# Clustered attention with two expert layers: who prepares the first two heads, and in which order

## What is computed

```python
q_assign = np.argmax(np.einsum('bhsd,hcd->bhsc', q_n, c_n), axis=-1)
k_assign = np.argmax(np.einsum('bhsd,hcd->bhsc', k_n, c_n), axis=-1)
mask = q_assign[:, :, :, None] == k_assign[:, :, None, :]
scores = scale * np.matmul(q, k.transpose(0, 1, 3, 2))
scores = np.where(mask, scores, -1000000000.0)
...
attn = attn / (np.sum(attn, axis=-1, keepdims=True) + 1e-09)
return np.matmul(attn, v).astype(np.float32)
```

## Time and profile before

| | us |
|---|---|
| median of 3 runs (839.62 to 842.99) | 840.84 |
| profiled execution | 838.19 |
| its span, first to last instruction | 836.4 |
| PE busy | 812.5 (97%) |
| DVE busy | 454.3 (54%) |
| ACT busy | 349.4 (42%) |
| POOL busy | 378.2 (45%) |

### The profile page before, as it was taken

One profiled execution on the slowest core, in us unless ns is written; L12 is line 12 of the kernel. 1 busy time (PEld: TensorE's weight loads), 2 busy tenths in 40 slices (PEclk: granted clock), 3 DMA queues, 4 the chain that ended last, 5 costly groups with the idle time before them and its releaser, 6 DMA issues.

```text
span 836.4 us, 13018 instructions
## 1 busy us (share of the span) xinstructions
PE 812.5 (97%) x4375; PEld 679.6 (81%) x4376; DVE 454.3 (54%) x685; ACT 349.4 (42%) x703; POOL 378.2 (45%) x323
## 2 busy tenths in 40 slices
PE   8999999999999899999999999999999999999995
PEld 4888898898898588888888888888888888888883
DVE  2969879879887779999877104531211121111110
ACT  1858678678687343334333443111212111121111
POOL 6997988988985255545545644000411011010001
PEclk8999999999999999999999999999999999999998
DMA  7444534534424287887767413300101000010001
GB/s 185 124 111 122 139 101 131 138 101 131 101 79 119 47 259 226 243 248 244 245 203 236 125 39 103 112 1 13 38 1 51 1 26 1 5 47 0 1 1 50
DMA packets 53114, 86.72 MB, mean 104 GB/s; under 512 B 22289, under 2 KB 24337, under 8 KB 53073
## 3 DMA queue, kind: packets, MB, share of 16 engines
q1 hardware_dynamic: 43920, 69.88, 29.3%
q0 software_dynamic: 3824, 11.29, 4.5%
q10 hardware_dynamic: 5328, 5.01, 1.8%
HBM read 73.29 MB, written 11.30 MB: 101 GB/s over the span
## 4 chain that ended last, share of the span: by engine, by line
PE 89%; POOL 5%; DVE 3%; issue 2%; DMA 1%; SPq 0%; ACT 0%; DVEq 0%; POOLq 0%
PE bank L1326 12%; PE bank L1328 12%; PE bank L1327 12%; PE bank L1419 8%; PE bank L1354 8%; PE bank L1228 6%; PE bank L1359 4%; PE bank L1423 4%; PE bank L1244 4%; PE bank L1212 3%; PE bank L1218 3%; PE bank L1246 3%; PE bank L1366 2%; PE bank L1257 2%; PE bank L1192 2%
## 5 line engine op out<-in xcount | busy, mean ns | idle before, releaser
L1159 DVE TENSOR_TENSOR ab_raw<-bank,a_sb 128x512 f32<-128x512 f32 x36 | 24.9, 691 | 195.2 <-PE bank L1328 189.3
L1007 DVE TENSOR_REDUCE neg_max<-bank 128x1 f32<-128x768 f32 x96 | 91.6, 954 | 40.5 <-PE bank L1218 39.6
L377 DVE TENSOR_TENSOR w_split<-stage,w_split 128x1024 fp32r<-128x1024 f32 x72 | 104.2, 1450 | 2.4
L761 ACT ACTIVATE pT_hi<-bank 128x384 fp32r<-128x384 f32 x192 | 84.9, 491 | 48.6 <-PE bank L1228 47.2
L373 DVE CAST w_split<-stage 128x1024 fp32r<-128x1024 f32 x68 | 66.0, 971 | 71.2 <-PE bank L1359 52.0
L978 DVE TENSOR_TENSOR pT_lo<-bank,pT_hi 128x384 fp32r<-128x384 f32 x192 | 97.5, 549 | 4.8 <-ACT pT_hi L761 4.8
L782 ACT ACTIVATE probs<-bank,neg_max 128x768 f32<-128x768 f32 x96 | 87.1, 908 | 11.6 <-DVE neg_max L1007 11.5
L655 POOL TENSOR_TENSOR hT_lo<-hT_raw,hT_hi 128x512 fp32r<-128x512 f32 x38 | 55.0, 1449 | 76.5 <-ACT hT_raw L830 76.0
L1228 PE MATMUL bank<-ident,probs 128*128 128x128 f32 x576 | 81.0, 275 | 1.8 <-ACT probs L782 1.1
L1419 PE MATMUL bank<-w_split,hT_hi 128*128 (+1 forms) x304 | 79.4, 403 | 0.5 <-issue 0.5
L886 ACT ACTIVATE a_sb<-bank 128x512 f32<-128x512 f32 x36 | 21.5, 598 | 139.0 <-PE bank L1328 139.0
(11 more groups left out here) (210 smaller groups left out, 1725.9 us busy)
## 6 DMA issues: line engine op xcount, KB each, us to landing
stage<-w SPq DMA_DIRECT2D x64, 512.0 KB
q_raw<-qT SPq DMA_DIRECT2D x32, 192.0 KB, 3.8
k_raw<-kT SPq DMA_DIRECT2D x32, 192.0 KB, 4.0
sorted_y<-y_sb ACTq DMA_DIRECT2D x19, 256.0 KB, 4.9
q_pair<-qT SPq DMA_DIRECT2D x8, 384.0 KB, 4.4
k_pair<-kT SPq DMA_DIRECT2D x8, 384.0 KB, 4.7
v_raw<-v_keys SPq DMA_DIRECT2D x16, 192.0 KB, 4.2
stage<-w_a SPq DMA_DIRECT2D x6, 512.0 KB
```

What stands on the lines that cost most here:

```text
L377: eng.tensor_tensor(dst[:, 1], stage[:, i % STAGES], dst[:, 0].bitcast(F32), ALU.subtract).then_inc(s_cv, 1)
L761: act.activation(pT_hi[:, half, part * GT:(part + 1) * GT, j * P:(j + 1) * P], pT_ps[part].rearrange("p (k q) -> p k q", q=P), ACT.Copy).t ...
L1007: dve.tensor_reduce(neg_max[:, qt % 2:qt % 2 + 1], scores[qt % 2][:, 0:S], AX_X, ALU.max, negate=True).then_inc(s_max, 1)
```

## The change

Only the work up to the first score of head 2 changes.

- ACT issues the four loads of head 0's rows, which SP issued before. Behind the square root ACT evaluates one exponential of a spare element and writes the identities of `back_w` from `ident`.
- `first_highs`: ACT writes the high parts `k_hl` and `q_hh` of heads 0 and 1, and for head 0 also the scaled q and the copy of k. `first_lows`: Pool keeps the low parts, and for head 1 the scaled q and the copy of k, on 64 partitions.
- Pool's iotas and selects stand ahead of its first wait for rows; the fills go to DVE, ahead of the centroids.
- The first pair's similarities go to two banks, six tiles each; DVE assigns the first half while PE multiplies the second, in two times five steps.
- PE transposes the one-hots twice, the second time shifted by two blocks (`one_hot` has two blocks more in front), so that head 0's rows come out in partitions 64 to 79 each time. ACT writes head 0's k mask and DVE its q mask straight to `k_hm` and `q_lm`; SP's mask DMAs for head 0 fall away, those for head 1 stay.
- Ahead of head 0's scores PE has 6 and 4 spins, where it had 9 and 14.
- Head 0's mask semaphore counts one pair less from then on; waits that are always met in the first pair are left out.

```diff
-        one_hot = sb("one_hot", [P, 4 * QT, 2 * C], BF16, att)
+        one_hot = sb("one_hot", [P, 2 + 4 * QT, 2 * C], BF16, att)
...
+        first_hot_T = bank[:, 6, :].bitcast(BF16)[:, 0:S]
+        first_sims = [bank[:, 7 - i, 0:2 * QT * C].rearrange("p (t c) -> p t c", c=C) for i in range(2)]
...
+        def load_rows(eng, g, slot):
+            for half in range(2):
+                rows = slice(half * D, half * D + D)
+                for raw, src in ((q_raw, qT), (k_raw, kT)):
+                    eng.dma_start(raw[rows, slot, :], src[bass.ds(g, 1)].rearrange("g d s -> (g d) s")).then_inc(s_qk[slot], 16)
...
             load_pair(0)
-            load_qk(0, 0)
             load_qk(1, 1)
...
             reload_pair(1)
-            mask(0, 0, 0)
             mask(1, 0, 1)
...
-            pool.memset(cen_pair[:, :, :, :], 0.0).then_inc(s_const, 1)
-            pool.memset(one_hot[:, :, :], 0.0).then_inc(s_const, 1)
             pool.iota(c_minus[:, :], pattern=[[1, C]], base=-C, channel_multiplier=0,
                       allow_small_or_imprecise_dtypes=True).then_inc(s_const, 1)
...
+            pool.wait_ge(s_set, 8)
+            pool.affine_select(out=tri[:, :], in_=tri[:, :], compare_op=ALU.is_ge, fill=0.0, base=0,
...
-            prepare(0, 0, 0)
-            prepare(1, 0, 1)
+            def first_lows(g):
+                q, k = q_raw[0:D, g], k_raw[D:P, g]
+                pool.wait_ge(s_khi, g + 1)
+                pool.tensor_tensor(k_hl[D:P, g], k, k_hl[D:P, g].bitcast(F32), ALU.subtract).then_inc(s_khl, 1)
+                pool.wait_ge(s_khl, g + 1)
+                pool.wait_ge(s_qs, g + 1)
+                pool.wait_ge(s_qhh, g + 1)
+                pool.tensor_tensor(q_lm[0:D, g], q, q_hh[0:D, g].bitcast(F32), ALU.subtract).then_inc(s_qlm, 1)
+                pool.wait_ge(s_qlm, g + 1)
+
+            pool.wait_ge(s_const, 17)
+            first_lows(0)
+            pool.wait_ge(s_qk[1], 64)
+            pool.wait_ge(s_khm, 1)
+            pool.tensor_tensor(k_hm[0:D, 1], k_raw[0:D, 1], one[0:D], ALU.mult).then_inc(s_khm, 1)
+            pool.wait_ge(s_qhh, 2)
+            pool.wait_ge(s_qs, 1)
+            pool.tensor_tensor(q_raw[0:D, 1], q_raw[0:D, 1], scale[0:D], ALU.mult).then_inc(s_qs, 1)
+            pool.wait_ge(s_khm, 2)
+            pool.wait_ge(s_qs, 2)
+            first_lows(1)
             split_v(0, 0, 0)
-            pool.memset(back_w[:, :, 0:D], 0.0).then_inc(s_const0, 1)
...
+            load_rows(act, 0, 0)
             act.wait_ge(s_csum, 1)
             act.activation(cen_n[:, 1:2], cen_n[:, 0:1], ACT.Sqrt).then_inc(s_csqrt, 1)
+            act.wait_ge(s_csqrt, 1)
+            act.activation(exp_spare[:, :], cen_n[:, 1:2], ACT.Exp, scale=0.0)
+            act.wait_ge(s_const, 1)
+            for half in range(2):
+                rows = slice(half * D, half * D + D)
+                act.activation(back_w[rows, :, 0:D], ident[rows, rows].unsqueeze(1).to_broadcast([D, G, D]), ACT.Copy).then_inc(s_bw, 1)
...
+            def first_highs(g):
+                act.wait_ge(s_qk[g], 64)
+                act.activation(k_hl[:, g], k_raw[:, g], ACT.Copy).then_inc(s_khi, 1)
+                act.activation(q_hh[:, g], q_raw[:, g], ACT.Copy, scale=float(D) ** -0.5).then_inc(s_qhh, 1)
+
+            first_highs(0)
+            act.wait_ge(s_qhh, 1)
+            act.activation(q_raw[0:D, 0], q_raw[0:D, 0], ACT.Copy, scale=float(D) ** -0.5).then_inc(s_qs, 1)
+            act.activation(k_hm[0:D, 0], k_raw[0:D, 0], ACT.Copy).then_inc(s_khm, 1)
+            first_highs(1)
...
             act.wait_ge(s_line, 4)
+            act.wait_ge(s_hotT, 1)
+            act.activation(k_hm[D:D + C, 0], hot_T[D:D + C, :], ACT.Identity, scale=mask_line[D:D + C, 0:1],
+                           bias=mask_line[D:D + C, 1:2]).then_inc(s_km0, 1)
             make_mask_rows(0)
...
+            for m, value in ((tri, 1.0), (before_e, 1.0), (rows_before_e, float(P)), (one_hot, 0.0), (cen_pair, 0.0),
+                             (ones, 1.0), (logits, 0.0)):
+                dve.memset(m[tuple([slice(None)] * len(m.shape))], value).then_inc(s_set, 1)
+            dve.memset(tile_thr[:, :, 0:1], -1.0).then_inc(s_set, 1)
...
             dve.tensor_scalar(cen_rows[:, :, :], cen_rows[:, :, :], cen_n[:, 7:8], None, ALU.mult).then_inc(s_cunit, 1)
-            dve.wait_ge(s_const, 5)
+            dve.wait_ge(s_const, 3)
+            dve.wait_ge(s_set, 8)
             dve.wait_ge(s_cT, 1)
-            for two in range(2):
-                rows = slice(two * D, two * D + D)
-                unit_T = bank[rows, 7, 0:P].rearrange("d (j two c) -> d j two c", two=2, c=C)[:, :, two, :]
-                for b in range(B):
+            for b in range(B):
...
-            for step in range(5):
-                assign(0, step)
+            for half in range(2):
+                n = 2 * QT
+                at = slice(half * n, half * n + n)
+                by_c = lambda v: v[:, at].unsqueeze(2).to_broadcast([P, n, C])
+                dve.wait_ge(s_sims0 if half == 0 else s_sims, 1)
+                dve.tensor_reduce(sim_max[:, at], first_sims[half], AX_X, ALU.max).then_inc(s_asgn, 1)
+                dve.wait_ge(s_asgn, 1 + 5 * half)
+                dve.tensor_tensor(sim_is_max[:, at, :], first_sims[half], by_c(sim_max), ALU.is_equal).then_inc(s_asgn, 1)
...
+                dve.tensor_tensor(one_hot[:, 2 + half * n:2 + half * n + n, 0:C], c_minus_ps[:, 0:n, :], by_c(first_idx),
+                                  ALU.is_equal).then_inc(s_asgn, 1)
+            dve.wait_ge(s_hotQ, 1)
+            dve.tensor_copy(q_lm[D:D + C, 0], first_hot_T[D:D + C, :]).then_inc(s_qm0, 1)
...
+            def first_similarities(half):
+                for t in range(QT):
+                    last = sim_rows(0, half * QT + t, first_sims[half][:, 2 * t:2 * t + 2, :])
+                last.then_inc((s_sims0, s_sims)[half], 1)
+
...
+            def first_hot_transposes():
+                pe.wait_ge(s_asgn, 10)
+                for out, back, done in ((hot_T, 2, s_hotT), (first_hot_T, 0, s_hotQ)):
+                    for t in range(QT):
+                        last = pe.transpose(out[:, t * P:(t + 1) * P],
+                                            one_hot[:, back + 4 * t:back + 4 + 4 * t, :].rearrange("p a c -> p (a c)"), ident_bf[:, :])
+                    last.then_inc(done, 1)
...
                     pe.wait_ge(s_qlm, g + 1)
                     pe.wait_ge(s_khm, g + 1)
-                    pe.wait_ge(s_mask[slot], (pp + 1) * 32)
+                    if slot == 1:
+                        pe.wait_ge(s_mask[1], (pp + 1) * 32)
+                    elif static(pp) and pp == 0:
+                        pe.wait_ge(s_qm0, 1)
+                        pe.wait_ge(s_km0, 1)
+                    else:
+                        pe.wait_ge(s_mask[0], pp * 32)
...
             pe.wait_ge(s_line, 6)
-            similarities(0, range(2 * QT))
-            spin(9)
-            hot_transposes(0)
-            spin(14)
+            pe.wait_ge(s_pair, 32)
+            pe.wait_ge(s_cTs, 2)
+            first_similarities(0)
+            first_similarities(1)
+            spin(6)
+            first_hot_transposes()
+            spin(4)
             over_pairs(pe, pair)
...
```

More of the change, by code:

```diff
@@ L416, in load_qk @@
             def load_qk(g, slot):
-                for half in range(2):
-                    rows = slice(half * D, half * D + D)
-                    sp.dma_start(q_raw[rows, slot, :], qT[bass.ds(g, 1)].rearrange("g d s -> (g d) s")).then_inc(s_qk[slot], 16)
-                    sp.dma_start(k_raw[rows, slot, :], kT[bass.ds(g, 1)].rearrange("g d s -> (g d) s")).then_inc(s_qk[slot], 16)
+                load_rows(sp, g, slot)
             def load_v(g, slot):
@@ new lines, in _ @@
+            pool.iota(row_no1[:, :, :], pattern=[[0, 1], [1, P]], base=1, channel_multiplier=0,
+                      allow_small_or_imprecise_dtypes=True).then_inc(s_const, 1)
+            pool.iota(place_no[:, :, :], pattern=[[P, T], [0, 1]], base=0, channel_multiplier=1,
+                      allow_small_or_imprecise_dtypes=True).then_inc(s_const, 1)
+            for m, pattern, step in ((row_no, [[0, 1], [1, P]], 0), (tile_row, [[0, 1], [P, TILES]], 0), (token_lane, [[0, 1]], 1),
+                                     (token_tile, [[1, T], [0, 1]], 0)):
+                pool.iota(m[tuple([slice(None)] * len(m.shape))], pattern=pattern, base=0, channel_multiplier=step,
+                          allow_small_or_imprecise_dtypes=True).then_inc(s_const, 1)
@@ L940, in _ @@
             dve.tensor_scalar(cen_rows[:, :, :], cen_rows[:, :, :], cen_n[:, 7:8], None, ALU.mult).then_inc(s_cunit, 1)
-            dve.wait_ge(s_const, 5)
+            dve.wait_ge(s_const, 3)
+            dve.wait_ge(s_set, 8)
             dve.wait_ge(s_cT, 1)
-            for two in range(2):
-                rows = slice(two * D, two * D + D)
```

(6 more changed lines are left out.)

97 lines of the change are left out of this document (44 added, 53 removed).

## The result

| | before | after |
|---|---|---|
| median, us (8 runs each) | 841.91 (838.67 to 843.87) | 835.12 (833.10 to 837.84) |
| profiled execution, us | 838.19 | 835.20 |
| its span, us | 836.4 | 833.5 |

The ratio is 0.9922, 95% interval 0.9898 to 0.9946: faster by 0.8%, 6.8 us between the medians. The two profiled executions differ by only 3.0 us. Both numbers need an explanation.

The account below looks back on a forecast made before the run. PE was taken to bound the kernel (97% busy), with Pool setting the pace up to head 2. First score 2.8 + wait 1.98 + clock 1.60 = 6.4 us, so 840.84 - 6.4 = 834.4 us, range 831.2 to 838.2.

Parts of the forecast that it names:

- the footing: Gain subtracted from the timed median 840.84 us, 2.65 above the profiled execution, rather than from the profiled 838.19.
- Term 1: Ahead of head 2: with Pool's queue shortened, PE's wait of 1.98 us goes.
- The spare time: At head 2, Pool was to be ready at least 4 us before PE needs it.
- Term 2: In head 2: PE stays busy from head 1, so the 1.60 us lost to the lower clock are gained.
- Term 3: First score of head 0: its second half starts at 17.2 instead of 20.02, 2.8 us gained (1.0 to 3.8).
- the start of the similarities: In the front, first pair: similarities start at 7.1 to 7.8, taken as 7.4, against 7.11 before.
- the pair's rows come late: Rival at the front: shared engines delay the first pair's rows, term 3 shrinks to 1.5, 835.7 us; chance 0.16.
- The steps of the assignment: DVE in the front: steps of 192 elements take 0.36 us each, five with gaps 1.95 us.
- Head 0's rows: Loads in the front: land not much later than 9.90; preparation done below 15 us, so not the bound.
- the signs of being wrong: Similarities past 8.5, ACT's mask activation past 18, clock 0.5 in head 0 or 1, PE wait over 1 us before head 3.
- Slower: the lower clock stays: Rival in heads 0 and 1: PE stays at 1.2 GHz, losing 0.48 us per us, 844.0 us; chance 0.06.

Follow-up runs that it names:

- constants alone: Kernel before with only Pool's constants moved ahead of its first wait, fills on DVE, back_w identities on ACT; 834.64 us, ratio 0.9933.
- before with more fillers: Kernel before with 26 instead of 14 filler spins on PE ahead of head 0's first score; 838.46 us, ratio 0.9974.
- rows on SP: Changed kernel with head 0's rows loaded by SP behind the first pair's rows instead of by ACT; 834.0 us, ratio 0.993.
- second profile of before: Kernel before, unchanged, profiled once more; 841.94 us, mean clock 0.986.
- the kernel with the gate weights late: Changed kernel with head 0's rows on SP, gate weights loaded behind the second pair's rows, 5 spins instead of 2 behind the centroid transpose; 836.65 us, ratio 0.9944.
- the changed kernel measured again: Changed kernel, unaltered, timed and profiled a second time; 835.19 us, ratio 0.993.
- front alone: Changed kernel with Pool's constants, fills and back_w put back on Pool, only the new front left; 834.51 us, ratio 0.9926.
- 16 fillers: Changed kernel with 16 spin matmuls instead of 2 behind the centroid transpose; 834.38 us, ratio 0.991.
- rows on SP and fillers: Changed kernel with head 0's rows on SP, 6 spins instead of 2 ahead of the similarities, 6 between the first score's halves; 834.42 us, ratio 0.9936.

## Why the prediction held, and where it did not

The forecast was 834.4 us (831.2 to 838.2), faster; measured 835.12. The direction is right and so are two of the three terms, but that the number is off by only 0.7 us is luck: the sum was 3.6 us too large (6.38 for the 2.79 of the profiles), and the footing was off by 2.9 us the other way (840.84 - 2.79 = 838.05 for 835.12).

- **Term 1, the wait ahead of head 2: right.** 1.98 us were foretold; the constants alone brought 1.98, the whole change 2.11. The spare time was 7.9 us, where "at least 4" was said. One step in its working is off: head 0 does not last to 33.79, which is the second score of head 1; head 1's first score stands at 29.94. The figure served as an upper bound only. And what Pool waited for at 29.19 was head 2's rows, not the scores of head 0.
- **Term 2, the clock in head 2: right.** 1.60 foretold, 1.55 in the profile, 1.61 with the constants alone, and 1.58 (17.91 - 16.33) in before with more fillers, where only PE came later and the wait was shorter.
- **Term 3, the first score: wrong in sign.** +2.8 foretold, -0.87 in the profile. The step that failed is the start of the similarities, 7.4, taken with the remark that a second queue brings little bandwidth: the pair landed at 10.64. The rival "the pair's rows come late" had this mechanism, with 7.4 to 9.5; an even share of the engines was not its worst case; head 0's loads were issued first and came ahead of the centroids as well, on which DVE starts at 4.44, 1.3 us later than before. By the rule cited from the Trainium skill, "DMA: Bandwidth & Descriptors", section "Queues, rings and completion order", a delay was to be expected, and the run agrees: 8.5 us from issue to landing beside ACT's loads, 3.9 with all on SP's queue. Of the 3.69 us by which the second half missed 17.2, this start is 3.33; about 1.0 of it is the late centroids (DVE is through with them at 8.39), the rest the pair's k. The steps from there on were right in sum, 10.16 us for 9.8: the similarities took 5.12 up to the first filler for 3.9, since they ran wholly at the lower level behind the wait of 3.28, and what stands behind them 5.04 for 5.9. The steps of the assignment took 0.36 each, as reckoned. Head 0's rows, which were not to come much later than at 9.90, let ACT begin only at 11.28, but did not set the time. With the rows on SP's queue 16.52 came for 17.2. Of the signs of being wrong that the prediction named two came, both from this step: similarities past 8.5 with the pair's load as releaser, and a wait of PE of over 1 us.
- **The footing: wrong, in the other direction.** The sum was taken from the median, 840.84, as if the 2.65 us between it and the profiled execution would stay. They did not: the changed kernel's profiled execution, 835.20, lies at its median. So those 2.65 us were no fixed amount around the kernel. The two other profiles of before, at 841.94 and 842.99, paid them for lower clocks in heads 0 and 1 and in the routing; that the change removes most of this from the timed executions is likely, not shown. By the profile's own footing the sum says 831.8; 835.20 came.
- **The rivals.** "Slower: the lower clock stays" did not come about in the profiles of the changed kernel, but the kernel with the gate weights late shows it, and two of the three profiles of before have it already. Its price was set somewhat too high: each us at half speed was to cost 0.48. In the second profile of before heads 0 and 1 took 50.74 - 19.41 = 31.33 us, with the constants alone 45.91 - 19.82 = 26.09; that is 5.2 us for some 14 us at the lower level (0.57 over 16 us), 0.37 each. In before this moved head 3 by only 1.27, because Pool kept PE at head 2 anyway; in the changed kernel Pool would not have hidden it.

What stays open: what decides in which executions the clock falls in the routing, why it does so where the front was quick, and why the constants alone, which leave the wait of 1.08 ahead of head 0, show a mean clock under 0.990 in only one execution of seven, and what the two slowest executions of the changed kernel measured again, with clocks of 0.995 and 0.996, lost their time to. Filling the first wait kept the clock up in heads 0 and 1 but not in the routing.

## What to carry to other kernels

Work that fits before an engine's first wait for data should be taken off the queue that a later stage waits for; here moving the constants alone gave all of the gain, the rebuilt front alone gave as much, and the two together no more. A load that is on the path to the first matmul should not share the DMA engines with one that is not, even if another engine's queue could issue that one sooner; in the profiles this cost 3 to 4 us of the first score (19.30 and 20.15 for 15.98), though the medians do not show it. And if the timed executions of a kernel scatter by more than the profile explains, look at their mean granted clocks, and profile a second and a third execution before a sum is put on the median.

## What the runs showed of the hardware

- 768 KB of the pair in 128 partitions landed 3.8 us (before), 3.9 us (rows on SP) and 4.5 us (constants alone) after the issue of their second half when the queue held only the two 32 KB loads of the centroids ahead, and after 6.5 to 8.5 us in the four profiles with four loads of 192 KB in 64 partitions on ACT's queue beside them (front alone 6.5, 16 fillers 7.2, changed 7.6 and 8.5).
- The granted clock of the windows does not show every slow stretch. In the kernel with the constants put back it reads 1.00 from 8 to 16 us, and yet the similarities there take 0.61 us a pair, 0.43 from start to start, as at 0.50 in the changed kernel; with the gate weights late, also at 1.00, it is 0.39 and 0.22. The lengths of like matmuls decide:

```profile
8.00:16.00 8.00, 7.22 (x30) 5.88 (x30) 3.91 (x15) 4.62 (x6) 4.90 (x3) 1.00 0.92 187
```

```profile
9.21 0.61 PE L1246 MATMUL bank<-cen_pair,k_pair 128*128 128x32 f32 x2
```

```profile
8.63 0.39 PE L1242 MATMUL bank<-cen_pair,q_pair 128*128 128x32 f32 x2
```

- TensorE at 1.00 fell to 0.50 behind idle times of about 2 us in thin work (2.40 us ahead of head 0 in the second profile of before; 1.88 and 0.43 in the kernel with the gate weights late). In the first it stayed there for some 14 us, in the second for some 17, although it was busy in all of that time (16.00 of 16.00, and 17.57 of 18.00 with the 0.43); behind the 1.98 of the earlier trace rows for 3.4. Behind 0.30 in before with more fillers it stayed at 1.00, and so it did behind 1.10 in head 1 of the changed kernel and 1.32 within head 0 with the rows on SP and fillers.
- The executions of the kernel before on one chip differ by up to 6 us (837.79 to 844.24), roughly in step with their mean granted clock (0.995 to 0.982). Those of the changed kernel measured again differ by as much (832.39 to 838.64) without following it (0.993 to 0.996).
